# POOL divides the probabilities by their row sum, instead of VectorE dividing a pair's outputs, in an attention-and-MLP kernel

## The reference

```python
scores = scale * q_rot @ k_rot.T              # per batch and head
scores = scores - max(scores, axis=-1)
attn = exp(scores)
attn = attn / (sum(attn, axis=-1) + 1e-09)
x = attn @ v                                  # heads side by side: 1152 x 512
h = x @ w_in;  g = h * sigmoid(h);  x = g @ w_out
h = x @ w_in2; g = where(h > 0, h, exp(min(h, 0)) - 1); out = g @ w_out2
```

## Time and profile before

| | us |
|---|---|
| median of 3 runs | 562.35 (562.2 to 563.34) |
| profiled execution | 561.98 |
| its span, first to last instruction | 560.2 |
| PE busy | 536.2 (96%) |
| PEld busy | 529.0 (94%) |
| DVE busy | 279.0 (50%) |
| ACT busy | 344.6 (62%) |
| POOL busy | 347.5 (62%) |

### The profile page before, as it was taken

One profiled execution on the slowest core, in us unless ns is written; L12 is line 12 of the kernel. 1 busy time (PEld: TensorE's weight loads), 2 busy tenths in 40 slices (PEclk: granted clock), 3 DMA queues, 4 the chain that ended last, 5 costly groups with the idle time before them and its releaser, 6 DMA issues.

```text
span 560.2 us, 9272 instructions
## 1 busy us (share of the span) xinstructions
PE 536.2 (96%) x3308; PEld 529.0 (94%) x3308; DVE 279.0 (50%) x503; ACT 344.6 (62%) x726; POOL 347.5 (62%) x287
## 2 busy tenths in 40 slices
PE   1888889999999999999999999999999999999997
PEld 1777889999999999999999999999999999999997
DVE  5788755633258762336563237884334440057400
ACT  4899777755467765557775457775555663366531
POOL 6989989659646565645655654454544666656652
PEclk9999999999999999999999999999999999999999
DMA  8676735365254353344434442334333434334440
GB/s 332 199 219 187 204 102 179 103 198 160 95 166 138 99 165 124 113 116 152 124 108 142 117 117 91 116 105 136 111 108 110 131 129 134 123 124 131 130 144 29
DMA packets 43229, 77.16 MB, mean 138 GB/s; under 512 B 5296, under 2 KB 12848, under 8 KB 43184
## 3 DMA queue, kind: packets, MB, share of 16 engines
q1 hardware_dynamic: 41456, 74.21, 42.8%
q10 hardware_dynamic: 1728, 2.36, 1.1%
HBM read 63.57 MB, written 2.36 MB: 118 GB/s over the span
## 4 chain that ended last, share of the span: by engine, by line
PE 92%; ACT 3%; DVE 3%; issue 1%; DMA 1%; SPq 0%; ACTq 0%; DVEq 0%
PE banks L914 71%; PE banks L879 6%; PE banks L849 5%; PE banks L833 3%; PE banks L835 3%; PE banks L858 1%; ACT prob L449 1%; DVE neg_max L619 1%; PE banks L881 1%; DMA k_raw<-k 1%; PE banks L892 1%; DVE head_out L656 0%; ACT q_raw L434 0%; ACT k_st L419 0%; DVE pt_lo L626 0%
## 5 line engine op out<-in xcount | busy, mean ns | idle before, releaser
L331 POOL TENSOR_TENSOR w_lo<-w_raw,w_hi 128x512 fp32r<-128x512 f32 x192 | 246.8, 1288 | 194.8 <-ACT w_hi L489 194.5
L489 ACT CAST w_hi<-w_raw 128x512 fp32r<-128x512 f32 x189 | 117.7, 624 | 45.1 <-PE banks L914 41.2
L914 PE MATMUL banks<-x_lo,w_hi 128*128 128x384 f32 x384 | 129.8, 338 | 1.4 <-DVE x_lo L661 0.7
L914 PE MATMUL banks<-g_lo,w_hi 128*128 128x384 f32 x384 | 129.3, 337 | 0.0
L914 PE MATMUL banks<-g_hi,w_lo 128*128 128x384 f32 x384 | 128.7, 335 | 0.0
L914 PE MATMUL banks<-x_hi,w_lo 128*128 128x384 f32 x384 | 128.7, 335 | 0.0
L914 PE MATMUL banks<-x_hi,w_hi 128*128 128x384 f32 x384 | 128.5, 335 | 0.0
L914 PE MATMUL banks<-g_hi,w_hi 128*128 128x384 f32 x384 | 128.5, 335 | 0.0
L619 DVE TENSOR_REDUCE neg_max<-banks 128x1 f32<-128x576 f32 x72 | 54.3, 754 | 70.8 <-PE banks L835 69.4
L501 ACT ACTIVATE act_buf<-banks 128x384 f32<-128x384 f32 x96 | 47.2, 492 | 58.0 <-PE banks L914 57.7
L914 PEld LDWEIGHTS banks<-x_lo,w_hi 128*128 128x128 f32 x384 | 72.1, 188 | 3.1 <-DVE x_lo L661 1.6
(11 more groups left out here) (75 smaller groups left out, 723.2 us busy)
## 6 DMA issues: line engine op xcount, KB each, us to landing
w_raw<-w SPq DMA_DIRECT2D x192, 256.0 KB, 2.6
q_raw<-q SPq DMA_DIRECT2D x11, 384.0 KB, 3.1
q_one<-q_raw SPq DMA_DIRECT2D x44, 96.0 KB, 2.6
k_raw<-k SPq DMA_DIRECT2D x7, 576.0 KB, 4.6
k_st<-k_raw SPq DMA_DIRECT2D x28, 144.0 KB, 2.5
v_raw<-v SPq DMA_DIRECT2D x8, 320.0 KB, 3.0
out<-act_buf ACTq DMA_DIRECT2D x12, 192.0 KB, 2.5
q_two<-q_raw SPq DMA_DIRECT2D x22, 96.0 KB, 2.3
```

The source lines that it names most:

```text
L331: nc.gpsimd.tensor_tensor(w_st[LO][:, slot, :], w_raw[:, slot, :], w_st[HI][:, slot, :].bitcast(F32), ALU.subtract).then_inc(w_lo_done, 1)
L489: nc.scalar.copy(w_st[HI][:, slot, :], w_raw[:, slot, :]).then_inc(w_hi_done, 1)
L914: last = nc.tensor.matmul(dst, w_st[wp][:, slot, m * P:(m + 1) * P], src[xp][:, tile, :], start=start and n == 0, stop=stop and n == 2)
```

## The change

For the tiles of chunks 1 and 2 (n from 24, 48 tiles), DVE adds and inverts the row sum of each tile by itself (`invert_tile`, two instructions on 128x2 and 128x1 elements), POOL multiplies the tile in `prob` in place with that inverse (`scale_tile`, one instruction on 128x576 elements, right behind `weight_lo` in POOL's round), and PE's transposition waits for POOL in place of ACT. The pairs p from 4 on (8 of 12) lose `invert_sums`, `widen_sums`, `spread_sums` and `scale_outputs`; `output_hi` waits for `add_outputs` instead. Chunk 0's heads keep the old way. The transposition of tile 48 and the value products of the later even heads no longer wait for `scale_outputs`. In the first woven round (n = 0), where tile 24 is scaled, `invert_tile(24)` stands behind `output_lo(3)` on DVE, and `scale_tile(24)` before the zeroing of the padding on POOL.

```diff
@@ pool
+            def scale_tile(n):
+                pool.wait_ge(exp_done, n + 1)
+                pool.wait_ge(tile_inverted, n - H * QN + 1)
+                nc.gpsimd.tensor_scalar(prob[:, n % 3, :], prob[:, n % 3, :], tile_inv[:, 0:1], None, ALU.mult) \
+                    .then_inc(scaled, 1)
...
                 if n + AHEAD < ALL_UNITS:
                     weight_lo(n + AHEAD)
+                if n == 0:
+                    scale_tile(H * QN)
+                if tile is not None and QN * i + tile + 1 < STEPS:
+                    scale_tile(QN * i + tile + 1)
@@ scalar
             def output_hi(p):
-                act.wait_ge(out_scaled, p + 1)
+                if p < 4:
+                    act.wait_ge(out_scaled, p + 1)
+                else:
+                    act.wait_ge(out_added, 2 * p + 2)
...
                 if j == 2 and not first:
-                    if i % 2 == 0:
-                        widen_sums(p - 1)
                     copy_out_lo(i - 1)
                 if i % H == H - 1 and j == 7:
-                    widen_sums(p)
                     copy_out_lo(i)
@@ vector
+            def invert_tile(n):
+                i, t, m = n // QN, n % QN, n - H * QN
+                dve.wait_ge(exp_done, n + 1)
+                nc.vector.tensor_reduce(tile_sum[:, :], row_sum[:, i // 2 % 2, t, i % 2, :], AXES.X, ALU.add) \
+                    .then_inc(sum_done, 1)
+                dve.wait_ge(sum_done, m + 1)
+                if m:
+                    dve.wait_ge(scaled, m)
+                nc.vector.reciprocal(tile_inv[:, :], tile_sum[:, :]).then_inc(tile_inverted, 1)
...
                     if n == 0:
                         add_outputs(i - 1)
-                    scale_outputs(p - 1)
+                        scale_outputs(p - 1)
                     output_lo(p - 1)
+                    if n == 0:
+                        invert_tile(H * QN)
...
+                if tile is not None and QN * i + tile + 1 < STEPS:
+                    invert_tile(QN * i + tile + 1)
                 if not beside:
                     continue
-                if i % H == H - 1:
-                    if j == 6:
-                        invert_sums(p)
-                    if j == 7:
-                        add_outputs(i)
+                if i % H == H - 1 and j == 7:
+                    add_outputs(i)
                 if not first:
-                    if i % 2 == 0 and j == 1:
-                        invert_sums(p - 1)
                     if j == (3 if i % H == H - 1 else 4):
                         add_outputs(i - 1)
-                    if i % 2 == 0 and j == 6:
-                        scale_outputs(p - 1)
@@ tensor
             def transpose_tile(n):
-                pe.wait_ge(exp_done, n + 1)
+                if n < H * QN:
+                    pe.wait_ge(exp_done, n + 1)
+                else:
+                    pe.wait_ge(scaled, n - H * QN + 1)
...
-                if i % 2:
+                if i % 2 or i > H:
                     pe.wait_ge(out_added, i)
...
                 else:
-                    hidden_unit(start, range(1))
-                    spread_sums(ahead // 2 - 1)
-                    hidden_unit(start, range(1, KT - 1))
+                    hidden_unit(start, range(KT - 1))
                     hidden_unit(start + 1, range(KT - 1))
...
-                        if j == 6 and i % 2 == 0 and u >= 8:
-                            spread_sums(i // 2 - 1)
```

More of the change, by code:

```diff
@@ L70, in build @@
         inv_wide = sb("inv_wide", [P, QN, 2, D])
+        tile_sum = sb("tile_sum", [P, 1])
+        tile_inv = sb("tile_inv", [P, 1])
         head_out = [sb(f"head_out{n}", [P, CT]) for n in range(2)]
@@ L90, in inv_rows @@
         def inv_rows(p):
-            return banks[:, 4 if p % 4 == 3 else PV_BANK, 0:CT]
+            return banks[:, 4 if p == 3 else PV_BANK, 0:CT]
         def scores(n):
@@ L167, in build @@
         eps_done, inv_done, inv_wide_done, row_done = sem("eps_done"), sem("inv_done"), sem("inv_wide_done"), sem("row_done")
+        sum_done, tile_inverted, scaled = sem("sum_done"), sem("tile_inverted"), sem("scaled")
         pv_done = sem("pv_done")
@@ L379, in _ @@
                 r = p + 2
+                tile = tile_at(i, j) if i < ITERS else None
                 if n + AHEAD < ALL_UNITS:
                     weight_lo(n + AHEAD)
+                if n == 0:
+                    scale_tile(H * QN)
+                if tile is not None and QN * i + tile + 1 < STEPS:
+                    scale_tile(QN * i + tile + 1)
                 if n < 2:
@@ L446, in exp_tile @@
                     act.wait_ge(end_transposed, n - 2)
-                if t == 0 and i % 2 == 0 and i >= 4:
+                if t == 0 and i % 2 == 0 and 4 <= i < 12:
                     act.wait_ge(eps_done, i // 2 - 1)
@@ L845, in transpose_tile @@
                     pe.wait_ge(pt_lo_done, n - 1 if n < H * QN else n)
-                if n in (H * QN, 2 * H * QN):
+                if n == H * QN:
                     pe.wait_ge(out_scaled, i // 2)
@@ L886, in spread_sums @@
                 pe.wait_ge(inv_wide_done, p + 1)
-                if p % 4 == 3:
+                if p == 3:
                     pe.wait_ge(pt_lo_done, QN * 2 * (p + 1))
```

## The result

The changed kernel takes 570.08 us (median of 4, 569.76 to 570.5) against 562.62 us for the kernel before beside it (562.2 to 563.34): a ratio of 1.0128, 95% interval 1.0113 to 1.0143. It is 7.5 us slower. The forecast was 561.3 us, no change, and the time lies outside the range, in the place that the third rival had put near 570.

The account below looks back on a forecast made before the run. PE, busy 96% of the span, was taken as the bound. Removed transpositions -2.64, two lost at chunk starts +0.66, new wait at tile 25 +0.96 gave -1.02 us: from 562.35 to 561.3 us, range 559.7 to 563.2.

Parts of the forecast that it names:

- the third rival: POOL's scale dearer than any POOL row; above 1.7 us PE waits at some 18 second tiles; near 570 us; chance 0.14.
- What the removed transpositions are worth: On PE, three transpositions of spread_sums removed eight times, 0.33 us each time, 2.64 us at most.
- the two at the chunk starts: At the starts of chunks 1 and 2 PE waits longer for x_lo instead; 0.66 us lost, 1.98 left.
- the weights' low parts hold: POOL's weight subtractions still come in time; unit 13's is 4.9 us ahead of use against 2.4 us added work.
- tile 25 waits: POOL does a weight subtraction first, so PE waits 0.96 us anew for the scale, between 0.84 and 1.58.
- Tile 24 at a dear price: The first scaled tile fits by 0.3 us; at a scale of 1.42 us PE would wait 0.36 us.
- the term for POOL's multiplication: POOL's 48 new multiplications of 128x576 taken at 0.8 us each, with 0.68 and 1.42 as the ends.
- the way from the exponential to POOL's start: DVE's inverse ready 0.41 us after the exponential, then the scale on POOL with nothing added between.
- tile 28, for which the step was worked out: Second tile of a head: 2.17 us between exponential and transposition, 1.26 needed, so 0.9 us to spare.
- the second rival: Break even: the scale costs 1.42 us, tiles 25, 24 and 28 wait, sum +0.2, 562.6 us; chance 0.22.

Follow-up runs that it names:

- e2: The changed kernel without any scaling, tiles of chunks 1 and 2 left undivided and PE transposing behind the exponential: 559.03 us, ratio 0.9944 to the kernel before.
- e1: The kernel before plus 28 spare POOL multiplications and copies in chunk 2's units, seven forms four times each: tensor by a column of scalars costs 1.73 us.
- e3: The changed kernel with POOL's scale on only 240 of 576 columns, all waits and queue places kept: 560.2 us, ratio 0.996 to the kernel before.
- e5: The changed kernel with the scale of tiles 24 and 25 alone cut to 144 of 576 columns: 568.95 us, ratio 1.0114 to the kernel before.
- e11: The kernel before plus spare work in chunk 2's units, seven times: four POOL products in a row with one DVE operation beside them; 582.24 us, not for comparison.
- e7: The kernel of e6 with tile 24's inverse before chunk 0's last outputs and tile 25's scale ahead of the weight's low part: 560.99 us, ratio 0.9971.
- e9: The kernel of e7 with DVE's output_lo of pair 4 moved from round 25 to round 30: 560.41 us, ratio 0.9963 to the kernel before.
- e6: The changed kernel with POOL's multiplication written as a two-tensor product, the inverse column repeated by stride zero: 562.71 us, ratio 0.9998 to the kernel before.
- e10: The kernel of e8 with tile 24's inverse and multiplication taken in round 0, directly behind its exponential: 560.05 us, ratio 0.9956 to the kernel before.
- e4: The changed kernel with the multiplication on DVE directly behind the reciprocal, none on POOL: 563.7 us, ratio 1.0025 to the kernel before.
- e8: The changed kernel with the multiplication on ACT, one round later, behind the evictions of the unit just ended: 560.45 us, ratio 0.9963 to the kernel before.

## Why the prediction was wrong

**Right.** What the removed transpositions are worth (0.33 us each predicted, 0.34 to 0.37 in e2) and that the two at the chunk starts bring nothing. That the weights' low parts hold (from 60 us on PEld waits 0.5 us for them in the changed kernel, 1.0 before). That tile 25 waits and why. Tile 24 at a dear price (0.64 us). And the third rival: it named the second tiles, a price from which they wait (1.7 us; 1.55 by the traces), and a time near 570.

**Wrong: the term for POOL's multiplication.** The step put it at 0.8 us with 0.68 and 1.42 as the ends; it is 1.73 us, beyond both. The choice rested on counting inputs: one tensor in, so between the cast and the select. e1 shows that this does not order POOL's forms: tensor by a constant 1.65, product of two tensors 1.43, the same product with a repeated column 1.15, copy 0.67 us. The row of a two-tensor product was taken for an upper end, and nothing in the trace made it one. The estimate of 0.86 us from the Trainium skill (GPSIMD Engine Reference, section 3.1) misses by half as well: at that section's 1.2 GHz, 1.73 us are 3.6 cycles for each of 576 columns, not 1.8, and the measurement decides. e3 shows that this term carries the verdict: with 0.885 us in its place the same kernel is 2.15 us faster than before. The range was drawn at 563.2 by giving the third rival 0.14; the evidence for that number, "nothing on POOL here with one input is beyond 1.5 ns an element", was one row of another operation.

**Wrong in size: the way from the exponential to POOL's start.** The sum had 0.41 us for the inverse and nothing from the inverse to POOL. At the usual tile, with POOL free, the inverse is there after 0.39 and POOL starts after 0.56, so a multiplication above about 1.55 us, and not 1.7, makes PE wait (an estimate: 2.17 - 0.56 - 0.05). At tiles 37, 40, 61 and 64, in the first units of the second MLP, DVE has one operation more for each unit; there the inverse takes 0.92 us, behind `probs_lo`, and PE waits 0.66 to 0.70. At tiles 31, 43, 46 and 52 the inverse is there after 0.38 to 0.46, and POOL's multiplication starts 0.62 to 0.95 us behind the exponential, right after a weight's low part. At tile 28, for which the step was worked out, PE waits 0.20. The step looked at one tile and spoke for 18.

**Missing: what a wait brings with it.** PE's 2.24 us of idleness was followed by 1.6 us lost at 1.2 GHz. In e5's trace, with 0.79 us in its place, the clock holds and PE is 3.1 us earlier at the next tile; e11 and the slowest run of e5 say that the fall does not follow such a wait each time, nor need it. And a DVE operation that reads two tensors from SBUF can be held up by POOL; the prediction used this for `x_lo` at the chunk starts (1.33 against 0.56 us), but did not ask what it would do with POOL busy for 20 us on end (e7, e9).

**Third rival in detail.** It reckoned 0.3 us at each of 17 second tiles for 2.0 us; the changed kernel, at 1.73, has 5.8 us there, unevenly: 1.54 at tile 34, 0.3 to 0.5 at eight others and at tile 69, next to nothing at the rest. It came to the right total with no loss from the clock in it, and at a price of 2.0 us. With the measured 1.73 its own steps give 1.9 at tile 25, 0.6 at tile 24, 0.8 at tile 28 and 17 times 0.02, which is 1.7 us over before, an estimate near 564. That it said 570 is luck in the size; its mechanism is what the runs show. The other way round, the price alone does not account for the 7.5 us in the prediction's terms: it needs the missed 0.17 and 0.5 us at the second tiles, POOL's queue at tile 34 and the clock as well.

## What to carry to other kernels

An operation that is in no row has no upper end. Before its price is put into a sum, ask from which price on the change turns to a loss (here 1.42 us by the second rival's sum, against a guess of 0.8; in e6 the change broke even at 1.15), and give that side the weight of not knowing; or measure the form first, since one run of spare instructions gives it in several spellings, and the spelling was worth 0.6 us an instance here. When an operation moves to an engine with idle time, its latency between producer and consumer counts and not the engine's share, and the queues that feed on that engine (here DMAs that wait for it) belong to the walk. The saving itself was sound: with the multiplication on ACT, whose durations did not spread beside POOL, the change gave 2.4 us (e10).

## What the runs showed of the hardware

- POOL, fp32, 128x576, SBUF to SBUF: copy 0.67, product with a repeated column 1.15, product of two tensors 1.43, tensor by a constant 1.65, tensor by a column of scalars 1.73 us (e1).
- DVE's tensor by a column, 128x576: 0.52 us alone and up to 1.53 (e4) or 1.64 us (e11) beside POOL; a maximum over 128x576 is 0.75 us beside POOL (e11) as it is for the kernel's own (0.75 us, reading PSUM); ACT's multiplication is 0.77 to 0.79 us at all 48 tiles (e8).
- A DVE subtraction of 128x384 with two inputs in SBUF took 9.16 and 9.17 us in two kernels whose POOL ran without a gap (e6, e7), 3.00 in e5 and 2.13 in e3, against 0.54 to 0.56 undisturbed.
- TensorE's granted clock went to 0.50 after 2.24 us of idleness in a stretch that was otherwise full, and stayed at 1.00 after 1.31 us at the same place (windows of e6) and after 2.03 and 2.04 us ahead of tile 34 (e6, e7). In e11 it fell after 2.12, 3.00 and 3.35 us and stayed at 1.00 after 3.05.
